# Attention in front of two MLP stages on one Trainium2 core: reordered PE steps, reciprocals spread by DMA, output scaled from SBUF

## What is computed

```python
# B, H, S, D = 4, 8, 576, 64
scores = (1 / 8) * q @ k.T                       # per head, 576 x 576
thresh = max(scores, axis=-1) - tau
scores = where(scores >= thresh, scores, -1e9)
attn = exp(scores - max(scores)); attn /= attn.sum(-1) + 1e-9
x = (attn @ v) laid out as 2304 tokens x 512
x = relu(x @ w_in) ** 2 @ w_out                  # d_ff = 2048
# top-1 router over 8 experts, each relu(x @ w1[e]) @ w2[e], scaled by gates
```

## Time and profile before

| | us |
|---|---|
| median of 3 runs | 1112.6 (1110.62 to 1115.22) |
| the profiled execution, its time | 1115.1 |
| its span, first to last instruction | 1113.4 |
| PE busy | 1042.4 (94%) |
| DVE busy | 664.1 (60%) |
| ACT busy | 554.3 (50%) |
| POOL busy | 432.9 (39%) |

### The profile page before, as it was taken

The page is one execution under the profiler, slowest core; times in us unless marked ns, Lnnn a source line. Parts: engine busy times, 40 slices in busy tenths (PEclk is TensorE's granted clock), DMA queues, the critical chain, the costliest instruction groups (busy, mean ns, idle before and its releaser), DMA issues. The chain is left out here.

```text
span 1113.4 us, 22407 instructions
## 1 busy us (share of the span) xinstructions
PE 1042.4 (94%) x8153; PEld 924.9 (83%) x8153; DVE 664.1 (60%) x1336; ACT 554.3 (50%) x854; POOL 432.9 (39%) x689
## 2 busy tenths in 40 slices
PE   7999999999989999999899989999379999999995
PEld 5778787787869999999899989999367777777774
DVE  5888787877855534343334333433567777777773
ACT  4777777777762311111111111111167888777772
POOL 4777777777750000000000000000147766667752
PEclk9999999999998999999999999999579999999998
DMA  4323223232203100000000000000782455511100
GB/s 107 80 60 82 53 66 80 63 81 51 53 2 115 39 20 1 25 1 20 3 25 1 20 2 24 1 20 1 277 322 112 166 197 183 190 38 39 39 28 22
DMA packets 76314, 75.40 MB, mean 68 GB/s; under 512 B 48815, under 2 KB 54959, under 8 KB 76210
## 3 DMA queue, kind: packets, MB, share of 16 engines
q1 hardware_dynamic: 72690, 63.49, 18.5%
q0 software_dynamic: 3520, 10.49, 2.8%
HBM read 64.52 MB, written 10.49 MB: 67 GB/s over the span
## 5 line engine op out<-in xcount | busy, mean ns | idle before, releaser
L820 ACT ACTIVATE r_buf<-h_ps 128x288 f32<-128x288 f32 x128 | 52.7, 412 | 348.2 <-PE h_ps L777 348.2
L884 DVE TENSOR_TENSOR r_buf<-r_buf 128x288 f32<-128x288 f32 x128 | 58.7, 459 | 244.4 <-ACT r_buf L820 244.4
L1156 POOL MEMSET ones<- 128x128 bf16 x1 | 0.2, 210 | 454.0 <-POOLq L637 454.0
L1322 ACT ACTIVATE w_hi<-w_experts 128x2048 fp32r x88 | 161.5, 1908 | 14.0 <-issue 14.0
L1093 DVE TENSOR_TENSOR w_lo<-w_experts,w_hi 128x2048 fp32r<-128x2048 f32 x66 | 149.5, 2292 | 28.0 <-ACT w_hi L1322 28.0
L777 PE MATMUL h_ps<-x_hi,w_in_hi 128*128 128x288 f32 x512 | 154.5, 302 | 6.6 <-DVE x_lo L878 3.5
L777 PE MATMUL h_ps<-x_hi,w_in_lo 128*128 128x288 f32 x512 | 151.9, 297 | 3.4 <-issue 3.4
L777 PE MATMUL h_ps<-x_lo,w_in_hi 128*128 128x288 f32 x512 | 152.5, 298 | 0.0
L796 PE MATMUL y_ps<-g_hi,w_out_hi 128*128 128x288 f32 x512 | 151.5, 296 | 0.3 <-DVE g_lo L890 0.3
L796 PE MATMUL y_ps<-g_hi,w_out_lo 128*128 128x288 f32 x512 | 151.3, 296 | 0.0
L796 PE MATMUL y_ps<-g_lo,w_out_hi 128*128 128x288 f32 x512 | 151.2, 295 | 0.0
(11 more groups left out here) (193 smaller groups left out, 2338.6 us busy)
## 6 DMA issues: line engine op xcount, KB each, us to landing
w_experts<-in_moe_w_dram SPq DMA_DIRECT2D x16, 2048.0 KB, 12.6
k_raw<-in_k_dram SPq DMA_DIRECT2D x32, 128.0 KB, 3.1
q_raw<-in_q_dram SPq DMA_DIRECT2D x32, 128.0 KB, 2.9
w_raw<-in_moe_w_in_dram SPq DMA_DIRECT2D x16, 256.0 KB, 3.2
v_nat<-in_v_dram SPq DMA_DIRECT2D x16, 256.0 KB, 2.6
y_T<-in_moe_w_out_dram SPq DMA_DIRECT2D x16, 256.0 KB, 2.7
y_rows<-y_row SPq DMA_DIRECT2D x16, 256.0 KB, 2.2
v_odd<-in_v_dram SPq DMA_DIRECT2D x16, 64.0 KB, 2.3
```

Of the source, the lines that this page charges most:

```text
L820: nc.scalar.activation(r_buf[f % 2][:], h_ps[f % 2][:, 0:HALF], ACT.Relu).then_inc(relu_done, 1)
L884: nc.vector.tensor_tensor(r[:], r[:], r[:], ALU.mult).then_inc(g_ops, 1)
L1156: nc.gpsimd.memset(ones[:], 1.0).then_inc(pool_set, 1)
L1322: nc.scalar.activation(group_of(w_hi, g), raw_group(buf, g), ACT.Copy).then_inc(hi_done, 1)
```

## The change

- **PE.** The scores of the next chunk are moved ahead of the transposes of set 2; these, and the keys, queries and ends, come last in a step. `broadcast_rinv` and the two spreading products in `output_tail` are gone. `output_main` no longer has the full-width product with `v_mix` (L392, 2 passes): it makes five pairs of 64-column products instead of four, of which the fifth uses the halves of `v_mix`. The tail output is made at c = 3 and not at c = 2. Partial tiles (64 rows of keys, of probabilities and of values) become full ones over zeros or neighbouring columns.
- **SP.** `spread_rinv` is new, at the head of each turn of the loop: wait for the reciprocals, write them to DRAM (1,152 single floats, transposed), wait until they landed, wait for `x_done`, and issue four DMAs that read them back with a broadcast into `rinv_bc`.
- **ACT.** `copy_rinv` and its tail are replaced by `copy_output` and `copy_output_tail`, copies of `o_ps` and of the tail of `m_ps` to `x_raw`, of the same shapes. Set 2 is copied out at the start of the next step, ahead of sets 0 and 1. `q_hi` moves to c = 2, ahead of sets 0 and 1.
- **DVE.** The two scalings out of PSUM become one over 128x576 from SBUF (`normalise`), a pair later. `reciprocal` moves from c = 0 to c = 1, between the two maxima. `k_lo`, `q_lo`, `ends_lo` are one step later and ahead of the masks.

```diff
 def spread_rinv(i):                     # new, on SP
+    rows = rinv_rows[i % 2]
+    sp.wait_ge(rinv_ready, i + 1)
+    sp.dma_start(rows.rearrange("n q -> q n"), rinv[:], allow_slow_non_contiguous=True).then_inc(rinv_out, 16)
+    sp.wait_ge(rinv_out, 16 * (i + 1))
+    if i >= 1:
+        sp.wait_ge(x_done, i)
+    for h in range(2):
+        part = slice(h * D, (h + 1) * D)
+        sp.dma_start(rinv_bc[part, 0:MAIN].rearrange("p (a c q) -> p a c q", a=1, c=LAST),
+                     rows.rearrange("(a n) q -> a n q", a=1)[:, h:2 * LAST:2, :]
+                     .rearrange("a (b n) q -> a b n q", b=1)
+                     .broadcast_to([D, 1, LAST, P])).then_inc(rinv_in, 16)
+        sp.dma_start(rinv_bc[part, MAIN:S], rows[CHUNKS - 1:CHUNKS, h * TAIL:(h + 1) * TAIL]
+                     .broadcast_to([D, TAIL])).then_inc(rinv_in, 16)
-            for i in range(PAIRS):
+            for i in range(PAIRS + 1):
+                if i >= 1:
+                    spread_rinv(i - 1)
                 if i + 2 < PAIRS:
                     load_rows(i + 2)
...
 output_main, PE
-                for kc in range(LAST):
-                    pe.matmul(o_ps[0:D, cols], v_nat[b][:, 0, kc, :], pt[:, kc, :], ...
-                    pe.matmul(o_ps[D:P, cols], v_odd[b][:, kc, :], pt[:, LAST + 1 + kc, :], ...
-                pe.matmul(o_ps[:, cols], v_mix[b][:], pt[:, LAST, :], start=False, stop=(c == LAST - 1), ...
+                for kc in range(QC):
+                    even = v_nat[b][:, 0, kc, :] if kc < LAST else v_mix[b][:, 0:D]
+                    odd = v_mix[b][:, D:2 * D] if kc == 0 else v_odd[b][:, kc - 1, :]
+                    pe.matmul(o_ps[0:D, cols], even, pt[:, kc, :], ...
+                    last = pe.matmul(o_ps[D:P, cols], odd, pt[:, LAST + kc, :], ...
...
 the step loop, PE
-            for step in range(STEPS * PAIRS + 3):
+            for step in range(STEPS * PAIRS + 4):
-                if c == 1 and i >= 1:
-                    broadcast_rinv(i - 1)
                 if 0 <= made[0] < PAIRS:
                     for s in range(2):
                         transposed_probs(*made, s)
-                if c == 0 and i + 1 < PAIRS:
-                    transposed_k(i + 1)
-                if 0 <= used[0] and used[1] < LAST:
+                if 0 <= used[0] < PAIRS and used[1] < LAST:
                     output_main(*used)
+                if c == 3 and i >= 1:
+                    output_tail(i - 1)
+                if step + 1 < STEPS * PAIRS:
+                    scores(*divmod(step + 1, STEPS))
                 if 0 <= made[0] < PAIRS and sets_in(made[1]) == 3:
                     transposed_probs(*made, 2)
+                if c == 0 and i + 1 < PAIRS:
+                    transposed_k(i + 1)
                 if c == 1 and i + 1 < PAIRS:
                     transposed_q(i + 1)
-                if 0 <= used[0] and used[1] == LAST:
-                    output_tail(used[0])
                 if c == 3 and i + 1 < PAIRS:
                     transposed_ends(i + 1)
-                if step + 1 < STEPS * PAIRS:
-                    scores(*divmod(step + 1, STEPS))
...
 the step loop, ACT
-            for step in range(STEPS * PAIRS + 3):
+            for step in range(STEPS * PAIRS + STEPS):
-                made = divmod(step - 2, STEPS)
-                if c == 1 and i >= 1:
-                    copy_rinv(i - 1)
+                made, earlier = divmod(step - 2, STEPS), divmod(step - 3, STEPS)
+                if 0 <= earlier[0] < PAIRS and sets_in(earlier[1]) == 3:
+                    evacuate(*earlier, 2)
+                if c == 1 and i + 1 < PAIRS:
+                    k_hi(i + 1)
+                if c == 2 and i + 1 < PAIRS:
+                    q_hi(i + 1)
+                if c == 4 and i >= 1:
+                    copy_output_tail(i - 1)
+                if c == 4 and i + 1 < PAIRS:
+                    ends_hi(i + 1)
                 if 0 <= made[0] < PAIRS:
                     for s in range(2):
                         evacuate(*made, s)
                 if i < PAIRS:
                     exponential(i, c, 0)
-                if c == 0 and i + 1 < PAIRS:
-                    k_hi(i + 1)
-                if 0 <= made[0] < PAIRS and sets_in(made[1]) == 3:
-                    evacuate(*made, 2)
-                if c == 1 and i + 1 < PAIRS:
-                    q_hi(i + 1)
                 if c == 2 and i >= 1:
-                    copy_rinv_tail(i - 1)
-                if c == 3 and i + 1 < PAIRS:
-                    ends_hi(i + 1)
+                    copy_output(i - 1)
                 if i < PAIRS and len(heads_in(c)) == 2:
                     exponential(i, c, 1)
...
 the step loop, DVE
+            for step in range(STEPS * PAIRS + STEPS + 1):
...
+                if i < PAIRS:
+                    maximum(i, c, 0)
+                if c == 1 and 1 <= i <= PAIRS:
+                    reciprocal(i - 1)
+                if i < PAIRS and len(heads_in(c)) == 2:
+                    maximum(i, c, 1)
+                if c == 1 and i + 1 < PAIRS:
+                    k_lo(i + 1)
+                if c == 2 and i + 1 < PAIRS:
+                    q_lo(i + 1)
+                if c == 4 and i + 1 < PAIRS:
+                    ends_lo(i + 1)
                 if 0 <= before[0] < PAIRS:
                     for h in heads_in(before[1]):
                         mask(*before, h)
+                if c == 0 and i >= 2:
+                    normalise(i - 2)
```

More of the change, by code:

```diff
@@ L372, in transposed_probs @@
                 else:
-                    last = pe.transpose(out[0:TAIL, 0:P], probs[c][:, MAIN:S], ident[:])
+                    last = pe.transpose(out[:, 0:P], probs[c][:, S - P:S], ident[:])
                 last.then_inc(probs_set, 1)
@@ L606, in _ @@
             ends_lo(0)
-            for step in range(STEPS * PAIRS + 4):
+            for step in range(STEPS * PAIRS + STEPS + 1):
                 i, c = divmod(step, STEPS)
@@ L610, in _ @@
                 if i < PAIRS:
-                    for h in heads_in(c):
-                        maximum(i, c, h)
-                if c == 2 and i >= 1:
-                    normalise_main(i - 1)
-                if c == 3 and i >= 1:
-                    normalise_tail(i - 1)
+                    maximum(i, c, 0)
[9 more added lines that the diff above has]
+                    ends_lo(i + 1)
                 if 0 <= before[0] < PAIRS:
```

140 lines of the change are left out of this document (61 added, 79 removed).

## The result

The changed kernel takes 1181.25 us (median of 4 runs, 1176.65 to 1185.27); the kernel before, run beside it, 1112.16 (4 runs, 1110.62 to 1115.22). The ratio is 1.0616, with a 95% interval of 1.0571 to 1.0662. I had forecast 1107 and a range of 1094 to 1118: the prediction was wrong in sign and size. The slower rival had the mechanism and the place right, and I had priced it at 4 to 14 us over the kernel before (1117 and 1127 against 1112.6) instead of 69.

The account below looks back on a forecast made before the run. PE was taken as the bound, busy 39.05 of 40.00 us. 15 periods x 0.5 = 7.6 us gained, 2.4 lost at the end, -5.2 against the median 1112.6: 1107 us, range 1094 to 1118.

Parts of the forecast that it names:

- The landing of the float write: SP's write of 1,152 single floats to DRAM: taken to land in 2.9 us, bounds 2.2 and 8.5.
- Rival 2: SP becomes late, POOL waits for w_raw at c = 0: 1117 at a 5.0 us landing, 1127 at 6.0; chance 0.15.
- The sum for SP: Reciprocals, write, issues and loads in SP's turn: weights land at 22.4, 3.2 into the next pair; POOL wants them near 3.6.
- The point of 4.0 us: SP's float write was to cost nothing up to a landing of about 4.0 us.
- PE's layout: One pair laid out on PE in the new order, with bank waits: period from 19.71 to about 19.2 us.
- Of the 3.0 us, some 2.5 come back as bank waits: PE, per pair: 3.0 us of work and waits removed, of which some 2.5 return as waits for a bank.
- the 0.72 us of the column pairs: PE, output_main: swapping the full-width product for a pair of passes saves a 0.18 us shape change in four chunks.
- The end: End of the attention stage, after the last reciprocals: last scaling +2.0 us, up to +7; put at +2.4 with clock.
- Rival 1: ACT keeps up at c = 2, only the 1.22 us bank loop binds: period 18.42, 1095.6 us; chance 0.20.
- Rival 3: POOL's cuts of chunk 1, delayed by masks and scaling, push exponentials at c = 2 by 0.5 us: 1115; chance 0.15.
- the forecast's own range: Whole kernel: the forecast's case alone spans 1102 to 1112 us, half of it counted as faster; chance 0.50.

Follow-up runs that it names:

- The probe: Kernel before, with a dead, waited-for write of five kinds in rotation at the head of each of SP's 16 turns; one run, 1118.39 us.
- before, with column pairs: Kernel before, with five pairs of 64-column products in output_main in place of four and a full-width one; 1111.96 us, ratio 0.997.
- 36 bytes, timed: Changed kernel with the reciprocals written as 128 pieces of 36 bytes, so the output is scaled by the wrong ones; 1102.42 us, ratio 0.9903.
- no reciprocals by DMA: Changed kernel without spreading of the reciprocals; the scaling uses a constant 0.01, so the division by the sums is missing; 1097.67 us, ratio 0.9854.
- rows of nine: Changed kernel with reciprocals written to DRAM as 128 rows of nine and broadcast so; the scaling picks every ninth float; 1108.09 us, ratio 0.9934.
- and the copy earlier: Rows of nine, with ACT's copy of the main output moved from mid c = 2 to the end of c = 1; 1105.85 us, ratio 0.99.
- and the split moved: Rows of nine with the earlier copy, and POOL's weight split moved out of c = 1 (now c = 0, 2, 3, 4); 1103.35 us, ratio 0.9894.
- rows of nine, scores last: Rows of nine, with PE's scores put back to the end of a step; 1111.36 us, ratio 0.9964.

## Why the prediction was wrong

**The landing of the float write** is the step that failed: "I take 2.9, since the nearest row has the same 4-byte pieces", with an upper bound of 8.5. It is 9.4 us in the mean and 10.46 at the end, above the bound too. The row behind the 2.9 was `tau_col`: 128 single floats to SBUF. The probe gives 2.9 to 4.3 us for 1,152 floats to SBUF, so the row fitted its own target. What I held equal, the size of the pieces, was the wrong likeness; the target and the neighbours made the difference. The upper bound scaled 0.7 us by the number of floats, and the number hardly matters (8.4 us for 512), so it was near the truth by chance.

**Rival 2** had the mechanism right: the place (`split_w` ahead of the biases of chunk 1) and the sign. The sum for SP was near as well, once it has the landing that came: 4.6 + 9.4 + 2.6 + 9.1 + 3.2 less a pair of 19.2 puts the weights at 9.7 in the next pair, 6.1 us after POOL wants them at 3.6. Seven of POOL's ten waits are 6.8 to 12.9 us, typically 7.3; in four of the seven the weights, issued 0.63 us ahead of a write, landed after 4.8 to 8.4 us instead of 3.2, which the sum did not have. I stopped the rival's price at landings of 5 and 6 us, 1117 and 1127, below my own upper bound of 8.5. The loss is 4.8 us a pair in the mean (23.96 against 19.2) and falls on every other pair. By issues and landing alone, without any wait for reciprocals, SP's turn is 22.07 us and longer than a pair. The share of 0.15 followed from the 2.9. The point of 4.0 us from which the landing was to cost anything was not tested; the versions with landings of 1.4 to 3.6 us already have pairs with late weights.

**PE's layout** was right. Without the DMA part the three starts agree within 0.05 us and the period within 0.03 (19.18 against the 19.21 of the layout). "Of the 3.0 us, some 2.5 come back as bank waits" holds for the sum, and one of its terms was not what I took it for: the 0.72 us of the column pairs is shared with the move of the scores. The same layout already counts shapes in the new order, so this error didn't reach the period.

**The end**: forecast +2.0 at 2.9 us and up to +7 at the upper bound (its own terms give 7.6); the last scaling came 15.5 us after the last reciprocals (386.15 to 401.61) instead of 5.8, +9.7. The forecast's own formula with the landing that was measured gives 2.0 + 10.46 - 2.9 = +9.6: again only that term was off. It makes 9.7 of the 69.7 us by which the MLP starts later.

**Rival 1** (ACT keeps up) didn't come: ACT is 1.08 us late at c = 3, as in the layout, and 0.5 us taken off its chain shortened a typical pair by 0.5. **Rival 3** (POOL) was hardly there: with ACT's lateness reduced, moving one split on POOL gave 0.1 us a pair.

**With a short landing** (mean 2.0 us, 1.57 at the end) the change takes 1102.42, inside the forecast's own range of 1102 to 1112. That is in part luck. The forecast's sum, with 1.3 us less at the end, says that the attention stage gets 6.5 us shorter; the MLP starts 5.3 us earlier. The other 7.1 us between the two profiled spans lie in the stages behind, where the code is the same and the sum has no term.

**The stages behind.** One trace of each kernel; "stops" are PE's idle times inside the first MLP that no releaser ends.

| kernel | MLP starts, us | from there to the end | stops: us, times |
|---|---|---|---|
| before | 335.69 | 777.7 | 6.5, 4 |
| before, with column pairs | 332.75 | 775.0 | 5.8, 4 |
| changed | 405.38 | 769.5 | 3.0, 2 |
| 36 bytes, timed | 330.44 | 770.6 | 3.3, 2 |
| no reciprocals by DMA | 327.38 | 769.4 | 3.1, 2 |
| rows of nine | 336.16 | 773.4 | 3.5, 2 |
| and the copy earlier | 334.20 | 771.5 | 3.4, 2 |
| and the split moved | 330.12 | 771.9 | 3.7, 2 |
| rows of nine, scores last | 337.40 | 773.6 | 3.4, 2 |

All five traces of the kernel before and of what was built on it have four stops and 773.2 to 777.7 us behind the start of the MLP; all nine of the changed kernel and of what was built on it have two stops and 768.7 to 773.6. So of what each of the nine gains on the kernel before, 4 to 9 us between the profiled executions are not from the attention stage. (The one of the kernel before lies 2.5 us above its median.) Around one stop of the kernel before (663 to 671 us) the granted clock also falls to 0.50, which makes it dearer. What the stops wait for, and why there are fewer, no run shows.

## What to carry to other kernels

A DMA that somebody waits for in the middle of a queue of issues is priced by the whole turn of that queue: add up every wait, issue and landing of a turn and hold it against the period. Do it again for every version that shortens the period; here, with a landing of some 2 us, late weights went with the loss of most of the 0.5 us a pair that a better order had gained. Take a landing from a row with the same target and the same layout in memory, not only the same size of piece; and if no such row exists and the sum turns on it, say how far beyond the bounds the rival's price goes. A transpose by DMA writes of single floats is dear in landing time, and moving the wait away doesn't make it free; leave the data in rows as it comes, and let the reader's access pattern do the transposing, which here cost DVE 1.12 us in place of 0.69 and brought the kernel from 6% slower to 0.7% faster than before. Compare the stage that was changed, and not only the total: by the traces that 0.7% is not from the attention stage, which first gets shorter with the edits on top (by 1.5 and 5.6 us). And look at single periods before a mean: the mean of 19.3 us hid pairs of 18.8 and of up to 22.5.

## What the chip showed that I had not expected

- 1,152 single floats that are neighbours in DRAM and come from different partitions land in 7.6 to 12.9 us; the same floats 64 bytes apart in 4.2 to 4.7, in SBUF in 2.9 to 4.3, as 128 pieces of 36 bytes in 1.4 to 3.6.
- Such a write holds up others: an issue on SP behind it took 4.63 or 4.70 us instead of 0.63, a load issued just ahead of it landed after 11.0 us instead of 3.2, and engines stopped for up to 3.8 us with no releaser in the kernel. With nobody waiting for their landings, 16 such writes still cost 20 us.
- A bias of one column on POOL took 0.30 us alone and 1.95 beside a mask and a strided scaling on DVE.
- Three times as many broadcast bytes, at a DMA share of 0.56 instead of the 0.29 without any, left a typical pair within 0.1 us of where it was (19.28 against 19.18).
- The same MLP and expert code took 768.7 to 777.7 us, and the difference went with what stood ahead of it: four stops of PE in the first MLP behind the old attention stage, two behind the new one.
